# Global scores of a batch in one block, and eight value tiles a head in place of nine

## What is computed

```python
k_all = np.concatenate([k_g, k_l], axis=2)
v_all = np.concatenate([v_g, v_l], axis=2)
out_g = np.matmul(sm(scale * q_g @ k_all.T), v_all)
s_ll = np.where(abs(pos[:, None] - pos[None, :]) <= 32, scale * q_l @ k_l.T, -1e9)
s_l = np.concatenate([scale * q_l @ k_g.T, s_ll], axis=-1)
out_l = np.matmul(sm(s_l), v_all)
x = (heads side by side, 2304 tokens x 512)
# then a soft mixture of 8 experts over x (phi, w1, w2),
# then h = x @ w_in; out = (h - tanh(h)) @ w_out
```

## Time and profile before

| | us |
|---|---|
| median of 3 runs | 319.38 (318.92 to 320.33) |
| the profiled execution, its own time | 318.87 |
| its span, first to last instruction | 317.1 |
| attention stage, to the first turning of tokens | 109.18 |

### The profile page before, as it was taken

One profiled execution on the slowest core, in us unless ns is written; L12 is line 12 of the kernel. 1 busy time (PEld: TensorE's weight loads), 2 busy tenths in 40 slices (PEclk: granted clock), 3 DMA queues, 4 the chain that ended last, 5 costly groups with the idle time before them and its releaser, 6 DMA issues.

```text
span 317.1 us, 7840 instructions
## 1 busy us (share of the span) xinstructions
PE 306.9 (97%) x2987; PEld 220.3 (69%) x2987; DVE 211.9 (67%) x443; ACT 139.0 (44%) x293; POOL 64.8 (20%) x62
## 2 busy tenths in 40 slices
PE   7999999999999999999998999999999999999994
PEld 4576777777777786233335888788888888888883
DVE  3887988888889556721258877566556666566572
ACT  1366766666566642111137554432334222532531
POOL 0543434434335001000008964000000000000000
PEclk9999999999999999999999999999999999999999
DMA  7999999999999969999999000030003000300202
GB/s 236 376 375 341 334 377 407 370 401 372 375 390 343 391 232 378 414 407 412 415 419 406 21 2 0 1 132 2 0 0 134 0 0 0 135 1 0 99 2 74
DMA packets 18032, 69.56 MB, mean 219 GB/s; under 512 B 4176, under 2 KB 5840, under 8 KB 14288
## 3 DMA queue, kind: packets, MB, share of 16 engines
q1 hardware_dynamic: 18000, 69.14, 57.7%
HBM read 64.41 MB, written 4.46 MB: 217 GB/s over the span
## 4 chain that ended last, share of the span: by engine, by line
PE 86%; DVE 7%; issue 5%; ACT 1%; POOL 1%; DVEq 0%; POOLq 0%
PE ps L846 20%; PE ps L849 20%; PE ps L550 6%; PE ps L595 5%; PE ps L821 5%; PE ps L746 4%; PE ps L777 4%; PE ps L587 3%; PE ps L566 3%; DVE sc L1101 3%; PE ps L606 2%; PE ps L541 2%; PE ps L560 2%; PE ps L581 2%; PE ps L658 1%
## 5 line engine op out<-in xcount | busy, mean ns | idle before, releaser
L849 PE MATMUL ps<-wlo,gg 128*128 128x512 f32 x204 | 80.5, 395 | 0.0
L846 PE MATMUL ps<-whi,gg 128*128 128x512 f32 x204 | 80.3, 394 | 0.0
L1307 DVE SCALAR_TENSOR_TENSOR nt<-uu,ps 128x512 f32<-128x512 f32 (+2 forms) x80 | 48.4, 607 | 47.3 <-ACT uu L1008 47.1
L1008 ACT ACTIVATE uu<-ps 128x512 f32<-128x512 f32 (+2 forms) x80 | 42.8, 537 | 84.0 <-PE ps L821 78.2
L457 POOL TENSOR_TENSOR sc<-sc,mx 128x640 f32<-128x640 f32 x32 | 40.1, 1253 | 53.5 <-DVE mx L1106 53.5
L1318 DVE TENSOR_TENSOR gg<-nt,ps 128x512 fp32r<-128x512 f32 (+2 forms) x80 | 47.9, 601 | 0.1
L846 PEld LDWEIGHTS ps<-whi,gg 128*128 128x128 f32 x204 | 38.4, 188 | 8.8
L849 PEld LDWEIGHTS ps<-wlo,gg 128*128 128x128 f32 x204 | 38.4, 188 | 8.0
L1101 DVE TENSOR_TENSOR sc<-ps,cst 128x640 f32<-128x640 f32 x32 | 26.2, 820 | 7.5 <-PE ps L550 5.9
L821 PE MATMUL ps<-cT,Pst 128*128 128x512 f32 (+2 forms) x80 | 28.9, 361 | 0.7 <-DVE Pst L1289 0.6
L595 PEld LDWEIGHTS ps<-vv,eT 128*64 128x64 f32 x512 | 18.7, 137 | 13.4 <-issue 11.0
(11 more groups left out here) (130 smaller groups left out, 384.6 us busy)
## 6 DMA issues: line engine op xcount, KB each, us to landing
w<-moe_w SPq DMA_DIRECT2D x11, 2048.0 KB, 11.2
vv<-v_t SPq DMA_DIRECT2D x8, 1170.0 KB, 7.7
w<-moe_w SPq DMA_DIRECT2D x14, 512.0 KB, 11.6
kT<-k_t SPq DMA_DIRECT2D x16, 416.0 KB, 6.3
out<-oo SPq DMA_DIRECT2D x17, 256.0 KB, 2.2
qT<-q_t SPq DMA_DIRECT2D x16, 256.0 KB, 7.3
win<-moe_w_in SPq DMA_DIRECT2D x4, 1024.0 KB, 16.6
wout<-moe_w_out SPq DMA_DIRECT2D x3, 1024.0 KB, 22.2
```

Source lines behind the costliest of these rows:

```text
L846: pe.matmul(o, g, hi, start=(c == 0), stop=False)
L849: mm = pe.matmul(o, g, lo, start=False, stop=(c == NC - 1))
L1008: nc.scalar.activation(uu[c % 2][:, 0:width], cols(h_bank(i, c), width), ACT.Square, scale=(1.0 / 3) ** 0.5).then_inc(square_ready, 1)
L1307: nc.vector.scalar_tensor_tensor(out=nt[c % 2][:, 0:width], in0=uu[c % 2][:, 0:width], scalar=1.0, in1=cols(h_bank(i, c), width), op0=ALU. ...
```

## The change

It does five things.

1. The scores of both global units (4 and 9) of a batch are computed in one block, at step 0 of the same batch, behind the weighing of unit 0. The eight heads are laid out so that head j of the first half takes columns 32j and head j of the second half columns 32(j ^ 1), with the row half j % 2 for both, into banks 0 and 1 and banks 2 and 3. The other blocks stand at steps 1, 3 (units 5 and 7) and 5, 7 (units 0 and 2 of the next batch).
2. DVE takes both global units in ahead of normalising unit 0, into two `scg`. It takes heads in four steps ahead, not five. Since the global scores come before those of units 5 to 8, `rank` gives each unit's place in the count.
3. The block of unit 4 ahead of the loop goes.
4. `vv` has eight tiles a head: the fifth even one goes. The last 32 keys of a global unit are weighed from rows 64 to 95 of the last odd tile; its last turned piece has 96 columns so that those probabilities land on those rows. It comes second in the order of tiles.
5. SP's loads get new gates and a new order, and the semaphores of the keys and queries are divided anew.

```diff
-        vv = [place("vv0", [P, 4, 9, D + 1], F32)]
+        vv = [place("vv0", [P, 4, 8, D + 1], F32)]
...
+        def rank(k):
+            return k if k < 5 else 5 if k == 9 else k + 1
+
+        def global_rows(qd, j):
+            return 32 * (j ^ qd)
...
-        SCORES_AT = {(u - AHEAD) % U: u for u in (0, 2, 4, 5, 7, 9)}
+        SCORES_AT = {5: 0, 7: 2, 0: 4, 1: 5, 3: 7}
...
-                sp.wait_ge(scores_ready, U * (i - 1) + GQ[pr // 2] + 1)
+                sp.wait_ge(scores_ready, U * (i - 1) + (6, 6, 8, 10)[pr])
...
-                sp.wait_ge(scores_ready, U * (i - 1) + (2, 4, 7, 9)[pr])
+                sp.wait_ge(scores_ready, U * (i - 1) + (2, 4, 8, 10)[pr])
...
             keys(1, 2)
+            keys(1, 3)
             queries(1, 2)
-            keys(1, 3)
             queries(1, 3)
...
                 queries(i + 1, 1)
+                global_queries(i + 1)
+                keys(i + 1, 2)
+                queries(i + 1, 2)
                 load_w1(sp, i - 1, w1_loaded, w1s[i - 1][:])
-                keys(i + 1, 2)
                 keys(i + 1, 3)
-                global_queries(i + 1)
+                queries(i + 1, 3)
                 values(i + 1, 0)
-                queries(i + 1, 2)
-                queries(i + 1, 3)
                 spread_global(i, 0)
...
                 if k in GQ:
-                    pe.wait_ge(qg_loaded, 16 * i)
-                    pe.wait_ge(masked_ready, U * i + k - 1)
+                    pe.wait_ge(global_loaded, 48 * i)
                 else:
...
+                pe.wait_ge(masked_ready, U * i + rank(k))
...
+                    for j in range(4):
+                        for qd in range(2):
+                            one(qd, j, 0)
+                    for qd in range(2):
                         for j in range(4):
-                            pr = 2 * (k // 5) + j // 2
...
+                            mm = one(qd, j, 1)
+                        mm.then_inc(scores_ready, 1)
...
-                    pe.transpose(cols(5, P, odd)[0:SG, :], e[:, 512:544], ident).then_inc(gprobsT_ready, 1)
+                    pe.transpose(cols(5, P, odd)[0:GR, :], e[:, SL + SG - GR:SL + SG], ident).then_inc(gprobsT_ready, 1)
...
-                    for c in range(5):
-                        if c == 4:
+                    for c in (0, 4, 1, 2, 3):
+                        if c == 3:
                             waits()
                         for j in range(4):
+                            r = slice(GR - SG, GR) if c == 4 else slice(0, P)
+                            v = vo[qd][r, j ^ qd, 3, :] if c == 4 else ve[qd][:, j ^ qd, c, :]
...
-            wake_for_scores(1, 4, cst)
-            scores(4)
...
-                r = SG if k in GQ else P
+                r = GR if k in GQ else P
...
+            def global_maxima(i):
+                for qd in range(2):
+                    k = GQ[qd]
+                    dve.wait_ge(scores_ready, U * i + rank(k) + 1)
+                    dve.wait_ge(probsT_ready, U * (i - 1) + k + 1)
...
+                for qd in range(2):
+                    dve.wait_ge(masked_ready, U * i + rank(GQ[qd]) + 1)
+                    nc.vector.tensor_scalar(gmx[qd][:, 1:2], gmx[qd][:, 0:1], -SCALE, None, ALU.mult).then_inc(gmax_ready, 1)
...
+                    if k == 0:
+                        global_maxima(i)
                     normalise(i, k)
-                    if k + 5 < U:
-                        maxima(i, k + 5)
-                    elif not last:
+                    if 1 <= k <= 4:
+                        maxima(i, k + 4)
+                    elif 5 <= k <= 8 and not last:
                         maxima(i + 1, k + 5 - U)
```

More of the change, by code:

```diff
@@ L66, in program @@
     U = 10
+    GR = P // 2 + SG
     GQ = (4, 9)
@@ L110, in program @@
         qgT = place("qgT", [P, 4, SG], F32)
-        vv = [place("vv0", [P, 4, 9, D + 1], F32)]
+        vv = [place("vv0", [P, 4, 8, D + 1], F32)]
         vg = [place("vg0", [P, 4, 4, D + 1], F32)]
         early = at[0]
-        vv.append(place("vv1", [P, 4, 9, D + 1], F32))
+        vv.append(place("vv1", [P, 4, 8, D + 1], F32))
         vg.append(place("vg1", [P, 4, 4, D + 1], F32))
-        ve = [v[:, :, 0:5] for v in vv]
-        vo = [v[:, :, 5:9] for v in vv]
+        ve = [v[:, :, 0:4] for v in vv]
+        vo = [v[:, :, 4:8] for v in vv]
         sc = [place(f"sc{n}", [P, 640], F32) for n in range(2)]
@@ L120, in program @@
         eT = [place(f"eT{n}", [P, 640], F32) for n in range(2)]
-        scg = place("scg", [P, SL + SG], F32)
+        scg = [place(f"scg{n}", [P, SL + SG], F32) for n in range(2)]
         mx = [place(f"mx{n}", [P, 4], F32) for n in range(2)]
-        gmx = place("gmx", [P, 2], F32)
+        gmx = [place(f"gmx{n}", [P, 2], F32) for n in range(2)]
         den = place("den", [P, 4], F32)
@@ L247, in program @@
         zeros_ready, memsets_done, rowmax_ready, c_repeated = (sem(n) for n in ("zeros_ready", "memsets_done", "rowmax_ready", "c_repeated"))
-        qg_loaded = sem("qg_loaded")
-        qk_loaded = [sem(f"qk_loaded{n}") for n in range(4)]
+        global_loaded = sem("global_loaded")
+        qk_loaded = [sem(f"qk_loaded{n}") for n in range(2)]
+        q_loaded = {n: sem(f"q_loaded{n}") for n in (2, 3)}
         v_loaded = [sem(f"v_loaded{n}") for n in range(2)]
@@ L519, in wait_scores @@
                 if k in GQ:
-                    pe.wait_ge(qg_loaded, 16 * i)
-                    pe.wait_ge(masked_ready, U * i + k - 1)
-                else:
-                    pe.wait_ge(qk_loaded[head_of(k)[0]], 32 * i)
-                    pe.wait_ge(masked_ready, U * i + k)
+                    pe.wait_ge(global_loaded, 48 * i)
+                else:
+                    pair = head_of(k)[0]
+                    pe.wait_ge(*((qk_loaded[pair], 32 * i) if pair < 2 else (q_loaded[pair], 16 * i)))
+                pe.wait_ge(masked_ready, U * i + rank(k))
             def seen_keys(pr, t):
@@ L530, in scores, with one @@
             def scores(k):
-                bank = scores_ps(k)
                 if k in GQ:
-                    for part in range(2):
-                        for j in range(4):
-                            pr = 2 * (k // 5) + j // 2
[L537 to L542, removed]
+                    def one(qd, j, part):
+                        pr = 2 * qd + j // 2
+                        r = slice(64 * (j % 2), 64 * (j % 2) + 64)
+                        own = kT[pr][r, 0:768].rearrange("r (b n) -> r b n", n=96)[:, :, 0:64]
+                        keys = kT[pr][r, 768:768 + SG] if part else own
+                        at = global_rows(qd, j)
+                        o = ps[at:at + 32, scores_ps(GQ[qd]) + part, 0:SG if part else 512]
+                        return pe.matmul(o, qgT[r, pr, :], keys, start=True, stop=True)
+                    for j in range(4):
+                        for qd in range(2):
+                            one(qd, j, 0)
+                    for qd in range(2):
+                        for j in range(4):
+                            mm = one(qd, j, 1)
+                        mm.then_inc(scores_ready, 1)
                 else:
@@ L612, in batch @@
                     u = SCORES_AT.get(k)
-                    if last and u is not None and u < AHEAD:
+                    if last and k >= AHEAD:
                         u = None
@@ L1092, in maxima @@
                     nc.vector.tensor_tensor_reduce(
[L1093 to L1107, removed]
@@ L1142, in batch @@
                         copy_tokens(0)
+                    if k == 0:
+                        global_maxima(i)
                     normalise(i, k)
-                    if k + 5 < U:
-                        maxima(i, k + 5)
-                    elif not last:
+                    if 1 <= k <= 4:
+                        maxima(i, k + 4)
+                    elif 5 <= k <= 8 and not last:
                         maxima(i + 1, k + 5 - U)
-            for k in range(5):
-                if k == GQ[0]:
-                    dve.wait_ge(const_loaded, 16)
+            for k in range(4):
                 maxima(1, k)
+            dve.wait_ge(const_loaded, 16)
             with dve.Fori(1, NB) as i:
@@ L1430, in attention_layout @@
     v = np.concatenate([v, np.zeros((NB, NH, P, D + 1), np.float32)], axis=2)
-    tiles = [v[:, :, P * c:P * c + P] for c in range(5)] + [v[:, :, 64 + P * c:64 + P * c + P] for c in range(4)]
-    v_t = np.stack(tiles, axis=2).reshape(NB, 2, 4, 9, P, D + 1).transpose(0, 1, 4, 2, 3, 5).reshape(NB, 2, P, -1)
+    tiles = [v[:, :, 64 * a + P * c:64 * a + P * c + P] for a in range(2) for c in range(4)]
+    v_t = np.stack(tiles, axis=2).reshape(NB, 2, 4, 8, P, D + 1).transpose(0, 1, 4, 2, 3, 5).reshape(NB, 2, P, -1)
     vg_t = with_one(v_g).reshape(NB, 2, 4, SG, D + 1).transpose(0, 1, 3, 2, 4)
```

41 lines of the change are left out of this document (25 added, 16 removed).

## The result

| | before | after |
|---|---|---|
| median of 8 runs, us | 319.5 (318.53 to 320.83) | 322.19 (321.38 to 322.75) |
| the profiled execution, its own time | 318.87 | 322.6 |
| its span | 317.1 | 320.7 |
| attention stage, to the first turning of tokens | 109.18 | 112.34 |

The ratio of the medians is 1.0093, interval 1.0075 to 1.011: slower by 0.9%. The forecast was 322.2. Of the 3.6 us between the two spans, 3.16 are in the attention stage; what follows it took 208.36 against 207.92.

A forecast was written before the change was run, and what follows sets the result against it. PE, with work for 97% of the span, bounds the kernel. Start -0.45 and +0.2, three periods +0.5, last batch +2.5 sum to +2.8: 321.7 on the profiled 318.87, 322.2 us for a median; range 319.3 to 325.7.

The forecast's parts named there:

- Global block: PE's global scores: two blocks of 1.06 become one of 1.3 us, bounds 1.06 and 2.1.
- two rounds of 0.44: In the global block, eight 512-column matmuls run four abreast in two rounds of 0.44, 0.88 us together.
- Eight tiles: Global weighings on PE: two more changes of array shape add 0.2 us each weighing, bounds 0 and 0.4.
- The chain: DVE mask, reduction, POOL, exp, ACT copy, then PE's turn: four steps ahead, it stalls turn(6) 0.6 us.
- Mask to turn: From the end of unit 6's mask on DVE to turn(6) on PE, through POOL and ACT: 3.77 us.
- Period: Whole attention batch: 25.2 us against 24.91; waits grow from 1.0 to 1.7, work falls 0.4.
- Last batch: Without score blocks in steps 5 to 8 the waits show bare: 22.0 us against 19.48, +2.5.
- Start: Before batch 1: unit 4's block goes, -0.45 us; keys of pairs 2 and 3 needed sooner, +0.2, bounds 0 and 1.
- the step that put step 0 at 14.1: At the start, ACT's copy of unit 0 ends at 14.01, so step 0 begins at 14.1 against 14.59: -0.45 us.
- Loads: Later key loads in the attention stage cost nothing; 1.04 MB less of values is on no PE path.
- After the stage: What follows the attention stage only moves with it: nothing.
- The faster rival: Attention batches: chain under 3.2 us or DVE's mask 0.6 earlier gives 24.5 a batch, 317.5 us; chance 0.14.

The follow-up runs named there:

- on four places: The changed kernel with the heads of both halves on the same columns 32j of the array, same number of instructions; 325.8 us, ratio 1.0198.
- without the weights: Four kernels with 16 MB of expert weights issued only behind the four batches; step 0 of batch 1 to tokens: before 94.59, after 97.66 us.
- nine tiles in the changed kernel: The changed kernel with nine value tiles a head again instead of eight; 322.3 us, ratio 1.0109.
- pairs, unit 0 first and nine tiles: The changed kernel with DVE masking and reducing both heads of a pair together, unit 0 normalised before the global reductions, and nine value tiles; 322.27 us, ratio 1.0089.
- The kernel with pairs: The changed kernel with DVE masking and reducing both heads of a pair right behind their score block, at steps 1, 3 and 5; 320.27 us, ratio 1.0035.
- pairs with unit 0 normalised first: The changed kernel with DVE taking both heads of a pair together and normalising unit 0 ahead of the two global reductions, eight tiles; 320.23 us, ratio 1.0035.
- the weights of that batch were held back: The kernel with DVE taking pairs, with the 2 MB load of w1's fourth expert held until the last batch's last scores; 321.35 us, ratio 1.0055.

## Why the prediction was right

- **The number.** Forecast +2.8. The medians are 2.7 apart (319.5 and 322.19), the profiled executions 3.7, the attention stages in them 3.16. That the median fell on 322.2 to a hundredth is luck; the mechanism and its steps, below, are what held.
- **Global block.** Forecast 1.3, bounds 1.06 and 2.1; it is 1.09, and 1.99 on four places. The two rounds of 0.44 held; the extra issues cost almost nothing, and the lower bound was the better value. The rule that I weighed against it (the Trainium skill, "TensorEngine Tiling (Array Packing)", Gotcha 1: row tiles can't access one PSUM bank at once) says nothing of time; read as a limit on speed, as I did, it would have the block at about 2.1. Here both row halves write each bank, on column strips of their own, and the eight run abreast: the measurement decides against the rule for this form.
- **Eight tiles.** Forecast 0.2 a weighing, measured 0.27. Block and weighings together make PE's work 8 x 1.75 + 2 x 1.68 + 4 x 1.25 + 1.09 = 23.45 a batch; the forecast had 23.5. Two sizes were off and cancelled, which was luck.
- **The chain.** From G, the end of the global block: scores(7) forecast at 7.22, measured 100.56 - 93.30 = 7.26; turn(6) 10.67 and 10.69; turn(7) 13.15 and 13.29; turn(8) 15.5 and 15.56; tokens 19.0 and 19.04. Mask to turn was 3.77 and 3.84. In the last batch turn(7) waited 0.81 (forecast 0.7) and turn(8) 0.48 (0.6). Two links ahead of these were off and cancelled. DVE began on the global scores 0.38 behind G, not at G (rows below), and its two reductions are 0.65 apart, not 0.77; so scores(5) began at 2.17, forecast 1.86, and PE waited 0.42 there rather than 0.1, and 0.34 ahead of scores(7) rather than 0.6.
```profile
93.68 0.72 DVE L1106 CUSTOM_DVE_ANT_0 scg<-ps,cst 128x544 f32<-128x544 f32 x1 [1.66 <-PE ps L548]
...
95.47 1.32 PE L564 MATMUL ps<-kT,qT 64*64 64x160 f32 x32
```
- **Period** 25.2 forecast, 25.26 measured: 23.45 of work and 1.8 of waits (forecast 1.7). **Last batch** +2.5 and +2.39, of which 0.30 is work (the block 1.09 for 1.06, unit 4's weighing 0.98 for 0.71) and 2.1 waits.
- **Start.** Forecast -0.25, measured +0.09: the step that put step 0 at 14.1 failed. It took ACT's copy of unit 0 to end at 14.01 as before; it ended at 14.63, behind an exp(1) that came at 13.16 rather than 12.54. This start moves from run to run: step 0 stood at 13.78 to 14.84 in the runs of the changed kernel and its variants, so the sign of this term means nothing.
- **Loads.** No block of scores waited for a transfer, as forecast. The 1.04 MB less, which I gave as worth nothing, I can't price: in after no transfer is late (97.66 with and without the weights), but with nine tiles in the changed kernel PE stood 0.45 ahead of late values in the last batch, and with pairs, unit 0 first and nine tiles 2.21.
- **After the stage.** Forecast nothing, measured 0.44 in the two profiled runs; over the kernels timed here it was 207.9 to 208.6, so this is within its spread.
- **The faster rival** was priced at 317.5 if the chain came 0.6 sooner. The kernel with pairs is that case: the periods became 24.2 to 24.6 (priced 24.5), and the whole 320.27, not 317.5. The price left out that the values then come late, and that a last batch without scores to hide behind keeps its waits (22.27, where the price had it at about 19.1).

## What to carry to other kernels

When a block of work is moved ahead of others on a full engine, lay out the partner engines' chain behind it link by link, in-order neighbours too (here a copy behind an exp that waits), and treat the last round of the pipeline by itself, since it has no next batch's work to cover the chain: most of the loss stood there. Count what a change saves on the bound engine only after asking which transfer has how much to spare; here a schedule shortened by 1 us a batch ran into values that land 10 us after their issue.

## What was not expected of the hardware

- **Idle cost the clock.** In the run with nine tiles and pairs, PE sat idle for 2.21 us, and 1.2 us after it had gone on the granted clock fell from 1.00 to 0.50, the lower of its two levels (1.2 against 2.4 GHz). Windows of that kernel, columns as in the earlier trace rows:
```profile
90.00:92.00 2.00, 0.74 (x6) 0.43 (x8) 0.01 (x1) 0.83 (x2) 0.76 (x1) 1.00 0.99 403
92.00:93.00 1.00, 1.00 (x24) 0.65 (x32) 0.34 (x2) 0.00 (x0) 0.00 (x0) 0.73 0.93 396
93.00:94.00 1.00, 1.00 (x16) 0.22 (x8) 0.42 (x1) 0.00 (x0) 0.00 (x0) 0.50 0.98 414
94.00:95.00 1.00, 1.00 (x27) 0.74 (x12) 0.19 (x1) 0.00 (x0) 0.00 (x0) 0.50 1.03 438
95.00:96.00 1.00, 1.00 (x6) 0.94 (x4) 1.00 (x3) 0.42 (x2) 0.00 (x0) 0.56 1.17 391
```
  The clock fell at 92.46 and rose at 95.88. The same kernel without the weights kept 1.00 and is the measure. The block took 2.00 (92.49 to 94.49) rather than 1.08, and the step behind it, with its wait, 2.40 (to 96.89) rather than 2.16: 1.16 that the clock cost. The weighing of unit 0 had begun 2.37 later behind its turn and taken 0.08 longer. Together that is 3.61, which is what its last batch lost (24.59 and 20.98): a transfer that came 2.4 us late cost 3.6. Idle of 1.02, 1.11 and 1.47 in other kernels left the clock at 1.00.
- **A releaser "issue" can be a transfer.** Five kernels idled ahead of one weighing, four with "issue" and one with another engine named, and in all five the last part of vg landed 0.09 us before it started.
- **Open:** the idle ahead of the turn of unit 5 in the last batch (0.63 to 1.11, in three kernels). All its semaphores were up in the trace. It went when the weights of that batch were held back and in the runs without the weights, so transfers have part in it; it was absent, too, in the run whose last batch was already 2.2 us late. The traces have a lead: a packet of 16 KB of the instruction queue (q8) ends 1.3 to 1.5 us ahead of that turn in these three (at 98.99, 98.57 and 100.83), and 2.6 to 4.6 ahead in the eight other kernels with one global block (after among them), none of which idles there. That points to instructions that come late, but the trace doesn't say whose they are, and no run tests it.
- No version here beat the kernel before. Of those with the global scores in one block the nearest, pairs with unit 0 normalised first, can't be told from it.
